# Head pairs of a windowed attention, re-timed between the products of a dense layer

## The chip, the cores and the metric

The kernel runs on one core of a Trainium2 chip. The metric is the device time of one execution in microseconds. Five instruction streams run side by side and meet only at semaphores: PE (matrix products), ACT (ScalarE), DVE (VectorE), POOL (GpSimd) and SP, which issues loads and stores. Each stream is executed in the order in which it is written. An instruction that waits therefore holds everything behind it on its own engine.

## The reference

```python
scores = scale * q @ k.T                      # B=4, H=8, S=768, D=64
keep = (key < 4) | ((0 <= row - key) & (row - key < 128))
a = softmax(where(keep, scores, -1e9));  x = (a @ v) as [3072, 512]
h = x @ w_in;  x2 = (h - tanh(h)) @ w_out     # 512 -> 2048 -> 512
logits = x2 @ w_gate + modality_bias[modality_id]
e = argmax(logits);  g = softmax(logits)[e]   # 8 experts
out = g * (relu(x2 @ w1[e]) @ w2[e])          # 512 -> 1024 -> 512
```

## The kernel before, in words

Every large product is made from two float16 parts of each operand, hi and lo: lo·hi + hi·lo + hi·hi, summed in PSUM. The hi part is written by ACT as a scaled copy, the lo part by DVE or POOL as the difference.

**Units.** The 3072 tokens are 8 chunks of 384. A *pair* r is one block of 128 query rows for two heads: 12 pairs a chunk, 96 in all. Three consecutive pairs (t = 0, 1, 2) belong to the same heads and form a group g; their results share one PSUM tile, `x_out`. The pair t = 0 of an even chunk has fewer keys (132 columns, not 260) and no values product of its own.

**The stages of a pair**, each a function that emits its part on each engine:

- `score_pair`: PE writes the scores of two heads into two banks `s_ps` (L571); DVE adds the mask, writes `probs` and takes the negated row maximum in the same pass (L582); ACT takes the exponential with the row sum (L589). `probs` is a ring of two pairs.
- `normalise`: DVE adds 1e-9 and inverts the row sums (L602, L603); ACT scales into `normed` (L609).
- `gather_sinks` (only t = 2): DVE copies the sink columns of the six normalised tiles into `sinks`.
- `transpose_probs`: PE transposes `normed` into the bank `pt_ps` (L641); ACT copies `pt_hi` (L646), DVE makes `pt_lo` (L650). `transpose_sinks` (only t = 2) sends the sinks through the same bank `pt_ps` (L664, L669, L673).
- `weigh_values`: PE adds the values products to `x_out` (L707), and for t = 2 the sinks' product (L709). The first of a group waits until `x_out` of the group before has been copied out by
- `split_x` (only t = 2): ACT `xt_hi` (L729), DVE `xt_lo` (L732).

**The dense layer.** For chunk m and block f of 16: `mlp_in` (PE, 12 products of 384 columns into the single bank `h_ps`, L752), tanh on ACT (L764), the gate on DVE (L773), then `g_hi` on ACT (L783) and `g_lo` on DVE (L793), and `mlp_out` (PE, 9 products of 512 columns into three banks, L808).

**The order.** `alone` first runs 14 pairs with nothing of the dense layer beside them, together with loads, the scaling and splitting of q, k and v (`conversions`, `prepare_alone`) and the splitting of the weights. Then come 8 windows w, one for each chunk of the dense layer, of 32 *slots* k. An even slot holds `mlp_in` of the next block, an odd one `mlp_out` of this block. Pairs are scored in even slots, inside `mlp_in` (`between`), by the table `plan_slots`. The later stages follow by their age in slots: `ago(2)` is the pair that was scored two slots ago. Before the change transposes come at age 2, inverse and normalising at age 1, sinks at age 3, the values products at age 3 (odd slot, t = 0 and 1) or 4 (even slot, t = 2), and `split_x` at age 5. The split of v for the next batch, scales and weight splits are called at given slots in `prepare`; the routing of the chunk before in `gate_slot`. It borrows the scores' bank, and whoever writes that bank next waits for its last reader (`claim_scores`).

After window 7 the experts' blocks run (L1858, L1909). The change does not touch them.

## Time and profile before

| | us |
|---|---|
| device time, median of three | 1101.09 (1100.54 to 1101.55) |
| the profiled execution's own time | 1097.37 |
| its span in the trace | 1095.8 |
| `alone`, to the first `mlp_out` | 0 to 97 |
| windows 0 to 7 | 97 to 801 |
| experts' blocks | 801 to 1096 |

The page gives for each engine its busy time as a share of the span. The stretches above are cut at the dense layer's products with `w_out`; the rows further down give the same for some stretches. PE's busy time contains its waits only where no product is under way, so the length of a stretch less PE's busy time is the time in which PE does nothing. The windows differ in work: windows 0, 2 and 4 carry the split of v for the next batch, window 0 also the last splits of the weights, and window 7 has no pairs.

### The profile page before, as it was taken

To read this page: it belongs to the slowest core of one execution; us is meant where nothing else is said; L and a number is where in the kernel's file an instruction comes from. 1 tells how busy PE (TensorE), PEld (TensorE's weight loads), DVE (VectorE), ACT (ScalarE), POOL (GpSimd) and SP (SyncE) were. 2 spreads that over 40 slices of the span, in tenths; PEclk is the share of its full clock that TensorE was granted. 3 is DMA by queue.
4 is the path that set the end of the run, shared out by engine and by line. 5 is a ranking of instruction groups with operands and counts; after the bars stand their busy time and mean duration, and the time that the engine had idled before them with its cause. 6 is when DMAs were issued, how large, how long until landed. Compare 5 with 4: busy or idle time off the path is not lost.

```text
span 1095.8 us, 23839 instructions
## 1 busy us (share of the span) xinstructions
PE 995.6 (91%) x7968; PEld 605.7 (55%) x7968; DVE 651.0 (59%) x2272; ACT 581.4 (53%) x1329; POOL 328.7 (30%) x462
## 2 busy tenths in 40 slices
PE   2647889999899999989999989999999999999996
PEld 1524445554455455545455545555477777677774
DVE  6565777657767757766766774655765334543331
ACT  3676687656667656655766664645532223532221
POOL 5675676111224311213321121011024223222222
PEclk9857999999999999999999999999999999999999
DMA  8710000200300211110030020014023411211111
GB/s 301 256 34 19 18 22 32 106 18 18 64 17 19 47 76 36 10 55 18 18 65 18 18 47 2 1 40 173 1 30 104 150 47 48 53 30 52 45 53 42
DMA packets 24375, 60.30 MB, mean 55 GB/s; under 512 B 9504, under 2 KB 9760, under 8 KB 22752
## 3 DMA queue, kind: packets, MB, share of 16 engines
q1 hardware_dynamic: 15392, 45.77, 14.2%
q0 software_dynamic: 5728, 13.43, 3.9%
q8 instruction: 45, 0.74, 0.3%
q10 hardware_dynamic: 3168, 0.02, 0.1%
q14 instruction: 42, 0.34, 0.1%
HBM read 45.35 MB, written 14.12 MB: 54 GB/s over the span
## 4 chain that ended last, share of the span: by engine, by line
PE 63%; DVE 14%; issue 9%; ACT 8%; DMA 3%; DVEq 1%; POOL 1%; ACTq 0%; POOLq 0%; SPq 0%
PE h_ps L752 17%; PE acc L808 14%; PE pt_ps L1858 4%; PE s_ps L1858 4%; PE acc L1909 4%; PE h_ps L1909 4%; PE pt_ps L641 4%; PE s_ps L571 2%; PE x_out L707 2%; ACT probs L589 2%; DVE g_raw L773 2%; DVE pt_lo L650 2%; ACT normed L609 2%; PE s_ps L859 2%; ACT pt_hi L646 1%
## 5 line engine op out<-in xcount | busy, mean ns | idle before, releaser
L808 PE MATMUL acc<-w_out_all,g_hi 128*128 128x512 f16 x768 | 228.4, 379 | 0.0
L752 PE MATMUL h_ps<-xt_hi,w_in_all 128*128 128x384 f16 x960 | 197.7, 329 | 11.5 <-DVE g_raw L773 11.5
L808 PE MATMUL acc<-w_out_all,g_lo 128*128 128x512 f16 x384 | 145.6, 379 | 3.0 <-DVE g_lo L793 2.7
L764 ACT ACTIVATE g_raw<-h_ps,batch_scale 128x384 f32<-128x384 f32 x120 | 69.7, 581 | 117.3 <-PE h_ps L752 113.4
L752 PEld LDWEIGHTS h_ps<-xt_hi,w_in_all 128*128 128x128 f16 x960 | 88.4, 100 | 71.3 <-issue 15.5
L793 DVE SCALAR_TENSOR_TENSOR g_lo<-g_raw,batch_scale,g_hi 128x384 f16<-128x384 f32 x128 | 90.4, 706 | 50.8 <-ACT g_hi L783 50.6
L808 PEld LDWEIGHTS acc<-w_out_all,g_hi 128*128 128x128 f16 x768 | 75.1, 98 | 80.3
L783 ACT ACTIVATE g_hi<-g_raw,batch_scale 128x384 f16<-128x384 f32 x128 | 78.3, 612 | 68.5 <-DVE g_raw L773 66.8
L101 POOL TENSOR_TENSOR tick<-tick 1x1 f32<-1x1 f32 x83 | 15.6, 189 | 314.3 <-DVE payload L931 128.1
L650 DVE TENSOR_TENSOR pt_lo<-pt_ps,pt_hi 128x512 f16<-128x512 f32 (+1 forms) x96 | 62.1, 647 | 68.9 <-ACT pt_hi L646 58.3
L752 PE MATMUL h_ps<-xt_lo,w_in_all 128*128 128x384 f16 x480 | 99.0, 329 | 0.0
L589 ACT ACTIVATE probs<-probs,neg_max 128x260 f32<-128x260 f32 (+1 forms) x192 | 92.0, 482 | 9.7 <-DVE neg_max L582 9.7
L582 DVE CUSTOM_DVE_ANT_0 probs<-s_ps,mask 128x260 f32<-128x260 f32 (+1 forms) x192 | 70.0, 401 | 45.1 <-issue 36.4
L646 ACT ACTIVATE pt_hi<-pt_ps 128x512 f16<-128x512 f32 (+1 forms) x96 | 53.6, 558 | 72.8 <-PE pt_ps L641 72.8
L609 ACT ACTIVATE normed<-probs,row_sum 128x260 f32<-128x260 f32 (+1 forms) x192 | 83.1, 480 | 11.0 <-DVE row_sum L602 10.9
L773 DVE SCALAR_TENSOR_TENSOR g_raw<-h_ps,batch_scale,g_raw 128x384 f32<-128x384 f32 x120 | 73.8, 615 | 23.3 <-ACT g_raw L764 21.6
L641 PE MATMUL pt_ps<-ident,normed 128*128 128x128 f32 x352 | 62.1, 298 | 17.1 <-ACT normed L609 10.2
L450 POOL TENSOR_TENSOR q_lo<-qk_raw,q_hi 128x384 f16<-128x384 f32 x31 | 28.3, 914 | 128.5 <-ACT q_hi L446 128.5
L1822 ACT ACTIVATE xg<-xg,x_scale 128x512 f32<-128x512 f32 x23 | 16.6, 722 | 93.6 <-DVE x_undo L1819 93.6
L752 PEld LDWEIGHTS h_ps<-xt_lo,w_in_all 128*128 128x128 f16 x480 | 47.4, 99 | 31.9 <-issue 1.3
L429 POOL TENSOR_SCALAR qk_raw<-qk_raw,qk_scale 128x384 f32<-128x384 f32 (+2 forms) x62 | 40.1, 659 | 75.7 <-DVE qk_scale L420 75.7
L641 PEld LDWEIGHTS pt_ps<-ident,normed 128*128 128x128 f32 x352 | 40.1, 148 | 39.4 <-issue 21.1
(315 smaller groups left out, 2093.9 us busy)
## 6 DMA issues: line engine op xcount, KB each, us to landing
qk_raw<-in_qk SPq DMA_DIRECT2D x31, 454.0 KB, 3.3
raw<-in_w SPq DMA_DIRECT2D x16, 512.0 KB, 8.4
v_raw<-in_v SPq DMA_DIRECT2D x4, 1536.0 KB, 8.2
x_tokens<-x SPq DMA_DIRECT2D x24, 256.0 KB, 4.7
w_in_all<-in_w_in SPq DMA_DIRECT2D x4, 1024.0 KB, 9.7
w_out_all<-in_w_out SPq DMA_DIRECT2D x4, 1024.0 KB, 9.3
x_tokens<-g_raw SPq DMA_DIRECT2D x1, 1024.0 KB, 12.2
vs_raw<-in_v SPq DMA_DIRECT2D x24, 4.0 KB
```

The costliest lines, as they stand in the source:

```text
L582: eng.tensor_tensor_reduce(out=probs[:, r % RING, j, cols], in0=s_banks[j][:, cols], in1=m, scale=-SCALE, scalar=3.0e38, op0=ALU.add, op1= ...
L589: eng.activation(x, x, ACT.Exp, bias=neg_max[:, r % RING, j:j + 1], scale=-1.0, accum_out=row_sum[:, r % RING, j:j + 1]).then_inc(q["exped ...
L609: eng.activation(normed[:, 2 * t + j, cols], probs[:, r % RING, j, cols], ACT.Copy, scale=total)\
L641: mm = eng.transpose(out[:, j, b - first, :], normed[:, 2 * t + j, b * KB:b * KB + P], ident[:])
L650: eng.tensor_tensor(at(pt_lo), out, at(pt_hi), ALU.subtract).then_inc(q["pt_lo_done"], 1)
L752: mm = eng.matmul(h_of(m, f), w16[0][:, f, x * DM + k * P:x * DM + (k + 1) * P], r[:, par, k, :], start=(i == 0), stop=(i == 3 * KD - 1))
L773: eng.scalar_tensor_tensor(g, h_of(m, f), batch_scale[:, b, 0:1], g, ALU.mult, ALU.subtract).then_inc(q["g_done"], 1)
L783: eng.activation(g_hi[f % 2][:], g, ACT.Copy, scale=batch_scale[:, b, 1:2]).then_inc(q["g_hi_done"], 1)
L793: eng.scalar_tensor_tensor(g_lo[f % 2][:], g, batch_scale[:, b, 1:2], g_hi[f % 2][:], ALU.mult, ALU.subtract)\
L808: mm = eng.matmul(acc[t][:, :], l[f % 2][:, t * P:(t + 1) * P], w16[1][:, f, x * DM:(x + 1) * DM], start=(f == 0 and i == 0), stop=(f == N ...
L1858: mm = eng.matmul(hid_ps[c][:, (f - 4 * c) * P:(f - 4 * c + 1) * P], w[:, k, f * P:(f + 1) * P], x[p][:, k * P:(k + 1) * P], start=(i == 0 ...
L1909: mm = eng.matmul(y_ps[bank][:, :], l[:, f * P:(f + 1) * P], rhs, start=(f == 0 and i == 0), stop=(f == KF - 1 and i == 2))
```

## The change

- **Values products** (`weigh_values`): the last argument goes; all three pairs of a group are done at age 4, at the end of an even slot, after `mlp_in`. None is left at the end of an odd slot.
- **Free slots** (`plan_slots`): in window 0 slots 8, 16, 24 (10, 20, 30 before), in the others 6, 14, 22, 30 (4, 10, 16, 26 before). With 14 pairs in `alone` each free slot then stands right behind a pair t = 2. The last pair is scored in slot 20 of window 6, not 22.
- **Odd slots on ACT**: `split_x` first, then `mlp_split` (`g_hi`), sinks, and `normalise` last. On DVE: gate, `split_x`, `normalise`, `g_lo`, sinks.
- **Routing** (`gate_slot`), but for window 7: transposes in slots 6, 10, 14 (4, 10, 16), logits two slots later, choice from 17 (20), rank from 22 (26).
- **Batch of v**: maxima in slots 1, 3, 7, 7, 9, 11 (0 to 5), scale in slot 15 (9), the six multiplications in 16 to 21 and the six splits in 17 to 22, one a slot (every second slot from 10 and 12), the sinks' multiplication in 23.
- **`conversions`**: the maxima of q and k at 6g−9 and 6g−7 (6g−10 and 6g−9), both odd, the scale with the second.
- **`alone`**: scores of the next pair are issued right after the transposes on PE, and right after `normalise` on DVE, ahead of v's maxima, scale chains and `split_x`. v's maxima leave the startup; v's splits and the sinks come one or two half-steps later. Values products all run two pairs behind.
- **`sink_halves`** on POOL waits in batch 1 for `qk_mult` instead of `w_lo1`.

```diff
-                if b == 1:
-                    eng.wait_ge(q["w_lo1"], 14)
-                if b >= 2:
+                if b:
                     eng.wait_ge(q["qk_mult"], 2 * (2 * HP * b + 1))
...
-        def weigh_values(E, eng, r, last):
+        def weigh_values(E, eng, r):
...
-            if E == "pe" and last == (t == TPC - 1) and not is_first(r):
+            last = t == TPC - 1
+            if E == "pe" and not is_first(r):
...
-            if k in (4, 10, 16):
...
+            late = g == NC - 2
+            turns = (4, 10, 16) if late else (6, 10, 14)
+            chooses, ranks = (20, 27) if late else (17, 22)
...
-                tops = (1, 1, 1) if g == 1 else (6 * g - 10, 6 * g - 9, 6 * g - 8)
-                splits = (3, 4) if g == 1 else (6 * g - 5, 6 * g - 3)
+                tops = (1, 1, 1) if g == 1 else (6 * g - 9, 6 * g - 7, 6 * g - 7)
+                splits = (2, 3) if g == 1 else (6 * g - 5, 6 * g - 3)
...
-            if i < 2:
-                v_tops(E, eng, 0, 2 * i + 2)
-                v_tops(E, eng, 0, 2 * i + 3)
-            if i == 1:
+            if i in (0, 2):
+                for blk in range(TPC):
+                    v_tops(E, eng, 0, TPC * (i // 2) + blk)
+            if i == 2:
...
-            if i in (1, 2, 3):
-                v_split(E, eng, 0, i - 1)
-            if i == 2:
+            if i in (2, 3, 4):
+                v_split(E, eng, 0, i - 2)
+            if i == 4:
                 sink_multiply(E, eng, 0)
-            if i == 4:
+            if i == 5:
                 sink_halves(E, eng, 0)
...
-                if k < NB2:
-                    v_tops(E, eng, b, k)
-                if k == NB2 and E == "dve":
+                for blk in {1: (0,), 3: (1,), 7: (2, 3), 9: (4,), 11: (5,)}.get(k, ()):
+                    v_tops(E, eng, b, blk)
+                if k == 11 and E == "dve":
                     spread(E, eng, v_spread(b))
-                if k == 10:
+                if k == 15:
+                    v_scales(E, eng, b)
+                if 16 <= k < 22:
+                    v_multiply(E, eng, b, k - 16)
+                if 17 <= k < 23:
+                    v_split(E, eng, b, k - 17)
+                if k == 23:
                     batch_scales(E, eng, b)
-                if 10 <= k < 22 and k % 2 == 0:
-                    v_multiply(E, eng, b, (k - 10) // 2)
-                if 12 <= k < 24 and k % 2 == 0:
-                    v_split(E, eng, b, (k - 12) // 2)
-                if k == 22:
                     sink_multiply(E, eng, b)
...
+            if E in ("pe", "dve"):
+                score_pair(E, eng, 0)
             for r in range(ALONE):
                 if E == "pe":
-                    stage(score_pair, E, eng, r)
                     stage(transpose_probs, E, eng, r - 1)
-                    stage(weigh_values, E, eng, r - 2, True)
+                    if r + 1 < ALONE:
+                        score_pair(E, eng, r + 1)
+                    stage(weigh_values, E, eng, r - 2)
...
                 if E == "dve":
-                    stage(score_pair, E, eng, r)
                     stage(gather_sinks, E, eng, r - 1)
                     stage(transpose_probs, E, eng, r - 1)
+                    normalise(E, eng, r)
+                    if r + 1 < ALONE:
+                        score_pair(E, eng, r + 1)
+                    stage(split_x, E, eng, r - 2)
+                    stage(transpose_sinks, E, eng, r - 1)
                 prepare_alone(E, eng, 2 * r)
...
-                    if k not in ((10, 20, 30) if w == 0 else (4, 10, 16, 26)):
+                    if k not in ((8, 16, 24) if w == 0 else (6, 14, 22, 30)):
...
                     if not even:
                         mlp_out(E, eng, w, f, between)
-                        stage(weigh_values, E, eng, ago(3), False)
                     else:
                         if nxt:
                             mlp_in(E, eng, *nxt, between)
-                        stage(weigh_values, E, eng, ago(4), True)
+                        stage(weigh_values, E, eng, ago(4))
...
                     else:
+                        stage(split_x, E, eng, ago(5))
                         if nxt:
                             mlp_split(E, eng, *nxt)
+                        stage(transpose_sinks, E, eng, ago(3))
                         stage(normalise, E, eng, ago(1))
-                        stage(transpose_sinks, E, eng, ago(3))
-                        stage(split_x, E, eng, ago(5))
```

Three places in the order of the instructions. In the changed kernel the same lines have numbers one or two lower.

PE at the start of window 2, before. `x_out` 128x384 is the sinks' product that ends a group, `x_out` 64x128 begins the next group.

```order
L709 MATMUL x_out<-pt_hi,vs_all 128x384
L808 MATMUL acc<-w_out_all,g_lo 128x512
L808 MATMUL acc<-w_out_all,g_hi 128x512 x2
L808 MATMUL acc<-w_out_all,g_lo 128x512
L808 MATMUL acc<-w_out_all,g_hi 128x512 x2
L808 MATMUL acc<-w_out_all,g_lo 128x512
L808 MATMUL acc<-w_out_all,g_hi 128x512 x2
L707 MATMUL x_out<-pt_lo,v_hi 64x128 x2
L707 MATMUL x_out<-pt_hi,v_lo 64x128 x2
L707 MATMUL x_out<-pt_hi,v_hi 64x128 x2
```

The same place now:

```order
L807 MATMUL acc<-w_out_all,g_lo 128x512
L807 MATMUL acc<-w_out_all,g_hi 128x512 x2
L751 MATMUL h_ps<-xt_hi,w_in_all 128x384 x4
L751 MATMUL h_ps<-xt_lo,w_in_all 128x384 x4
L569 MATMUL s_ps<-k_hi,q_lo 128x260 x2
L569 MATMUL s_ps<-k_lo,q_hi 128x260 x2
L569 MATMUL s_ps<-k_hi,q_hi 128x260 x2
L639 MATMUL pt_ps<-ident,normed 128x128 x4
L751 MATMUL h_ps<-xt_hi,w_in_all 128x384 x4
L706 MATMUL x_out<-pt_lo,v_hi 64x128 x2
L706 MATMUL x_out<-pt_hi,v_lo 64x128 x2
L706 MATMUL x_out<-pt_hi,v_hi 64x128 x2
```

Before, the first product of the next group stands one `mlp_out` behind the end of the last group. Now a whole slot of `mlp_in` (with its scores and transposes) and more stands between them, and the product comes behind an `mlp_in`.

DVE in `alone`, at the pairs 10 and 11, before. `pt_lo` is of pair 10, `row_sum` of pair 11, `qk_exp` to `qk_scale` is the scale chain of a group of q and k.

```order
L650 TENSOR_TENSOR pt_lo<-pt_ps,pt_hi 128x2x256
L412 TENSOR_SCALAR qk_exp<-qk_top 128x1
L414 TENSOR_SCALAR qk_exp<-qk_exp 128x1
L412 TENSOR_SCALAR qk_exp<-qk_top 128x1
L414 TENSOR_SCALAR qk_exp<-qk_exp 128x1
L416 TENSOR_SCALAR qk_half<-qk_exp 128x1
L418 TENSOR_SCALAR qk_half<-qk_half 128x1
L419 TENSOR_SCALAR qk_scale<-qk_half 128x1
L420 TENSOR_SCALAR qk_scale<-qk_scale 128x1
L602 TENSOR_SCALAR row_sum<-row_sum 128x1
```

The same place now; `probs` is of pair 12.

```order
L648 TENSOR_TENSOR pt_lo<-pt_ps,pt_hi 128x2x256
L600 TENSOR_SCALAR row_sum<-row_sum 128x1
L601 RECIPROCAL row_sum<-row_sum 128x1
L600 TENSOR_SCALAR row_sum<-row_sum 128x1
L601 RECIPROCAL row_sum<-row_sum 128x1
L578 MEMSET tick 1x1
L580 ISA probs,neg_max<-s_ps,mask 128x260
L580 ISA neg_max 128x1
L580 ISA probs,neg_max<-s_ps,mask 128x260
L580 ISA neg_max 128x1
L401 TENSOR_REDUCE qk_top<-qk_raw 128x1
L412 TENSOR_SCALAR qk_exp<-qk_top 128x1
```

The chain of eight small operations stood between `pt_lo` and the inverse; it now stands behind the scores of the next pair, together with one of the maxima (`qk_top`).

ACT in window 0 where v is split (`v_hi`), before:

```order
L507 ACTIVATE v_hi<-v_raw 128x4x2x64
L783 ACTIVATE g_hi<-g_raw,batch_scale 128x384
L609 ACTIVATE normed<-probs,row_sum 128x260 x2
L669 ACTIVATE pt_hi<-pt_ps 128x384
L357 ACTIVATE w_in_all<-w_in_all,w_scale 128x512
L446 ACTIVATE q_hi<-qk_raw 128x384
L646 ACTIVATE pt_hi<-pt_ps 128x2x256
L764 ACTIVATE g_raw<-h_ps,batch_scale 128x384
L589 ACTIVATE probs,row_sum<-probs,neg_max 128x260 x2
L507 ACTIVATE v_hi<-v_raw 128x4x2x64
```

The same place now:

```order
L507 ACTIVATE v_hi<-v_raw 128x4x2x64
L446 ACTIVATE q_hi<-qk_raw 128x384
L644 ACTIVATE pt_hi<-pt_ps 128x2x256
L763 ACTIVATE g_raw<-h_ps,batch_scale 128x384
L587 ACTIVATE probs,row_sum<-probs,neg_max 128x260 x2
L507 ACTIVATE v_hi<-v_raw 128x4x2x64
L782 ACTIVATE g_hi<-g_raw,batch_scale 128x384
L607 ACTIVATE normed<-probs,row_sum 128x260 x2
L357 ACTIVATE w_out_all<-w_out_all,w_scale 128x512
L507 ACTIVATE v_hi<-v_raw 128x4x2x64
```

Before, ten instructions lie from one `v_hi` to the next, the two included. Now three splits of v stand in these ten rows.

## Rows read from the trace of the kernel before

**Rows 1.** Page, part 1: busy time, share of the span and instructions of each engine.

```profile
PE 995.6 (91%) x7968; PEld 605.7 (55%) x7968; DVE 651.0 (59%) x2272; ACT 581.4 (53%) x1329; POOL 328.7 (30%) x462
```

**Rows 2.** Busy time by stretch: stretch, length, each engine's busy us (instructions), clock, DMA.

```profile
0.00:97.00 97.00, 48.92 (x387) 30.96 (x388) 55.94 (x257) 54.67 (x142) 60.59 (x87) 0.79 0.48 172
97.00:195.00 98.00, 86.82 (x599) 46.02 (x597) 72.32 (x244) 72.90 (x170) 63.70 (x73) 1.00 0.07 21
195.00:282.00 87.00, 84.80 (x569) 46.61 (x568) 58.55 (x227) 53.63 (x137) 16.21 (x20) 1.00 0.16 45
282.00:376.00 94.00, 87.10 (x599) 47.90 (x597) 66.81 (x243) 59.21 (x145) 29.56 (x34) 1.00 0.14 30
...
801.00:1096.00 295.00, 280.08 (x3135) 208.27 (x3133) 119.78 (x343) 89.49 (x148) 81.92 (x152) 1.00 0.20 61
```

**Rows 3.** Waits of PE, 97 to 195 us: total us, times, longest us.

```profile
PE x_out L707 <- issue: 5.0, 3, 2.5
PE h_ps L752 <- DVE g_raw L773: 2.8, 4, 1.1
PE pt_ps L641 <- DVE pt_hi L673: 2.5, 4, 0.9
```

**Rows 4.** Waits of PE, 195 to 731 us.

```profile
PE x_out L707 <- issue: 10.6, 9, 2.2
PE h_ps L752 <- DVE g_raw L773: 7.1, 18, 0.9
PE pt_ps L641 <- DVE pt_hi L673: 4.4, 9, 0.6
```

**Rows 5.** Timeline of PE, 286 to 293 us: start, us, instruction, [idle before, releaser].

```profile
286.33 0.63 PE L641 MATMUL pt_ps<-ident,normed 128*128 128x128 f32 x4 [0.50 <-DVE pt_hi L673]
...
289.84 0.59 PE L808 MATMUL acc<-w_out_all,g_hi 128*128 128x512 f16 x2
292.67 0.25 PE L707 MATMUL x_out<-pt_lo,v_hi 128*64 128x128 f16 x2 [2.23 <-issue]
```

**Rows 6.** Timeline of DVE, the same stretch.

```profile
292.01 0.56 DVE L732 SCALAR_TENSOR_TENSOR xt_lo<-x_out,xt_hi 128x384 f16<-128x384 f32 x1 [0.56 <-ACT xt_hi L729]
```

**Rows 7.** Waits of ACT, 18 to 89 us.

```profile
ACT normed L609 <- DVE row_sum L602: 9.8, 8, 2.0
...
ACT probs L589 <- DVE neg_max L582: 5.2, 6, 1.6
```

**Rows 8.** Timeline of DVE, 75 to 78 us.

```profile
75.70 0.14 DVE L412 TENSOR_SCALAR qk_exp<-qk_top 128x1 int32<-128x1 int32 x1
...
77.14 0.14 DVE L602 TENSOR_SCALAR row_sum<-row_sum 128x1 f32<-128x1 f32 x1
```

**Rows 9.** Timeline of POOL, 27 to 30.4 us.

```profile
27.46 1.15 POOL L534 TENSOR_TENSOR vs_all<-vs_raw,vs_all 32x512 f16<-32x512 f32 x1 [0.43 <-ACT vs_all L524]
28.71 0.70 POOL L492 TENSOR_SCALAR v_raw<-v_raw,v_scale 128x512 f32<-128x512 f32 x1
29.37 0.94 POOL L450 TENSOR_TENSOR k_lo<-qk_raw,k_hi 128x396 f16<-128x396 f32 x1
```

**Rows 10.** Timeline of PE, 30 us.

```profile
30.36 0.23 PE L571 MATMUL s_ps<-k_hi,q_lo 64*128 64x132 f16 x2 [0.76 <-POOL k_lo L450]
```

**Rows 11.** Timeline of DVE, 16.7 us.

```profile
16.72 0.29 DVE L331 TENSOR_REDUCE row_top<-acc 128x1 f32<-128x128 f32 x1 [0.95 <-PE acc L324]
```

**Rows 12.** Timeline of ACT, 322 us.

```profile
322.31 0.62 ACT L507 ACTIVATE v_hi<-v_raw 128x512 f16<-128x512 f32 x1
```

**Rows 13.** Line 793 on DVE, 97 to 195 us, then 195 to 282 us: ns min/median/max.

```profile
L793 DVE SCALAR_TENSOR_TENSOR g_lo<-g_raw,batch_scale,g_hi x16: 619/1039/1504, 101.7 to 191.7; 128x384 f16<-128x384 f32 x16
...
L793 DVE SCALAR_TENSOR_TENSOR g_lo<-g_raw,batch_scale,g_hi x16: 617/618/619, 196.3 to 279.3; 128x384 f16<-128x384 f32 x16
```

**Rows 14.** Timeline of POOL, then DVE, 323 us.

```profile
323.00 1.16 POOL L510 TENSOR_TENSOR v_lo<-v_raw,v_hi 128x512 f16<-128x512 f32 x1 [9.03 <-ACT v_hi L507]
...
323.46 1.11 DVE L793 SCALAR_TENSOR_TENSOR g_lo<-g_raw,batch_scale,g_hi 128x384 f16<-128x384 f32 x1 [0.67 <-ACT g_hi L783]
```

More of the change, by code:

```diff
@@ L943, in gate_slot @@
         def gate_slot(E, eng, g, k):
-            if k in (4, 10, 16):
-                gate_transpose(E, eng, g, (k - 4) // 6)
-            if k in (6, 12, 18):
-                gate_logits(E, eng, g, (k - 6) // 6)
-            if 20 <= k < 25:
-                gate_choose(E, eng, g, (k - 20,))
-            at = 27 if g == NC - 2 else 26
-            if at <= k < at + 4:
-                gate_rank(E, eng, g, (k - at,))
+            late = g == NC - 2
+            turns = (4, 10, 16) if late else (6, 10, 14)
+            chooses, ranks = (20, 27) if late else (17, 22)
+            if k in turns:
+                gate_transpose(E, eng, g, turns.index(k))
+            if k - 2 in turns:
+                gate_logits(E, eng, g, turns.index(k - 2))
+            if chooses <= k < chooses + 5:
+                gate_choose(E, eng, g, (k - chooses,))
+            if ranks <= k < ranks + 4:
+                gate_rank(E, eng, g, (k - ranks,))
         def prepare_expert(E, eng, k):
@@ L1128, in startup @@
             conv(E, eng, 0, 0, 1)
-            v_tops(E, eng, 0, 0)
-            v_tops(E, eng, 0, 1)
             for s in range(2):
@@ L1170, in prepare_alone @@
                 weight_gram(E, eng, 0, i - 4)
-            if i in (4, 6, 8):
-                v_multiply(E, eng, 0, i // 2 + 1)
-            if i in (5, 7, 9):
-                v_split(E, eng, 0, (i + 1) // 2)
+            if i in (6, 8, 10):
+                v_multiply(E, eng, 0, i // 2)
+            if i in (7, 9, 11):
+                v_split(E, eng, 0, (i - 1) // 2)
             if i == 8:
@@ L1224, in before_slot @@
                 gate_slot(E, eng, w - 1, k)
-            if w % 2 == 0 and w < NC - 2 and k == 9:
-                b = w // 2 + 1
-                if E == "pe":
-                    spread(E, eng, v_spread(b))
-                v_scales(E, eng, b)
+            if w % 2 == 0 and w < NC - 2 and k == 15 and E == "pe":
+                spread(E, eng, v_spread(w // 2 + 1))
         def stage(work_on, E, eng, r, *more):
@@ L1235, in alone @@
         def alone(E, eng):
+            if E in ("pe", "dve"):
+                score_pair(E, eng, 0)
             for r in range(ALONE):
                 if E == "pe":
-                    stage(score_pair, E, eng, r)
                     stage(transpose_probs, E, eng, r - 1)
-                    stage(weigh_values, E, eng, r - 2, True)
+                    if r + 1 < ALONE:
+                        score_pair(E, eng, r + 1)
+                    stage(weigh_values, E, eng, r - 2)
                 if E == "act":
-                    stage(score_pair, E, eng, r)
+                    score_pair(E, eng, r)
                     stage(transpose_probs, E, eng, r - 1)
@@ L1255, in alone @@
                     stage(transpose_sinks, E, eng, r - 1)
-                    stage(weigh_values, E, eng, r - 1, False)
                 if E == "act":
                     stage(transpose_sinks, E, eng, r - 1)
-                    stage(normalise, E, eng, r)
-                if E == "dve":
-                    stage(normalise, E, eng, r)
-                    stage(split_x, E, eng, r - 2)
-                    stage(transpose_sinks, E, eng, r - 1)
+                    normalise(E, eng, r)
                 prepare_alone(E, eng, 2 * r + 1)
@@ L1323, in window @@
                             mlp_gate(E, eng, *nxt)
+                        stage(split_x, E, eng, ago(5))
                         stage(normalise, E, eng, ago(1))
@@ L1327, in window @@
                         stage(transpose_sinks, E, eng, ago(3))
-                        stage(split_x, E, eng, ago(5))
                 if w == NC - 1:
```

1 line of the change is left out of this document (removed).

## The prediction

> **What bounds the kernel now.** I read the page first, then busy time by stretch, then what PE waited for in each stretch, then the timelines around the longest waits. PE is busy for 995.6 us of the span [rows 1]. The stretches split the rest [rows 2]: `alone` has 97 − 48.9 = 48.1 us in which PE does nothing, window 0 98 − 86.8 = 11.2, window 1 2.2, window 2 6.9, and the experts' part, which no edit reaches, 14.9. So there are two kinds of place. In the windows PE is the bound and only its waits can be won. In `alone` PE is idle half the time, and a chain that runs from DVE to ACT and back sets the pace of the pairs.
>
> PE's waits in the windows with pairs are three kinds [rows 3, 4]: before the values products 5.0 + 10.6 = 15.6 us, before transposes (the bank `pt_ps` is still read for the sinks) 2.5 + 4.4 = 6.9, and before `mlp_in` (the single bank `h_ps`) 2.8 + 7.1 = 9.9. The first is put down to "issue", so I looked at its longest. PE's last `mlp_out` product starts at 289.84, then PE stands for 2.23 us until 292.67 [rows 5]; DVE's `xt_lo` of the group before ends at 292.01 + 0.56 = 292.57 [rows 6]. The wait is the one for `x_out` to be copied out.
>
> **The values products and the free slots, in the windows.** At age 4, and with a free slot behind each third pair, the first product of a group comes at age 8 counted from the scores of the pair that ended the group before, while `split_x` is written at age 5. Three slots lie between, and the pt parts of a pair are made at age 2. I take all 15.6 us off. The sinks' transposes go through `pt_ps` at age 3, and the transposes that used to follow at age 4 now find a free slot there in steady state. I take the 6.9 us off too. PE's work is the same, only its place moves. At the bank `h_ps` the count of PE instructions between one `mlp_in` and the next stays the same for a pair (values before `mlp_out` instead of behind it), so the 9.9 us stay. Sum of what goes: 22.5 us.
>
> What comes new in the windows:
>
> - v's scale in slot 15: PE's spread writes the scores' bank, and the logits of slot 16 may write it only when DVE has read it. That read is 0.29 us in the one place that I looked at [rows 11], but it stands in DVE's slot behind the gate, `g_lo` and the sinks. I take 0.7 us late, in windows 2 and 4 (window 0 has no routing): 1.4 us. From below it is 0, if DVE is ahead; from above 2.2, the longest wait of PE in these windows [rows 4], each time.
> - The transposes of the routing in slot 10 stand in a slot with scores, in six windows. Their copy on ACT has two thirds of an `mlp_in` to finish before the scores need the bank. I take 0, at most 0.6 each (about a `v_hi` of ACT, which copies as many elements [rows 12]).
> - The six splits of v come one a slot in windows 0, 2 and 4. ACT does 0.62 us for each [rows 12], POOL 0.70 for the multiplication [rows 9] and 1.16 for the difference [rows 14]. The 18 splits are the same work, but in a slot pair ACT now has 1.24 us of it, not 0.62. ACT is busy 74% of window 0 (72.9 of 98) and 63% of window 2 (59.2 of 94) [rows 2], so the surplus fits in windows 2 and 4 on average and hardly in window 0, which has the weights as well. I take 0.6 us a slot pair for three slot pairs, 1.8, in window 0 and half of that in each of windows 2 and 4: 3.6 us together. From below 0 (all hidden), from above each split holds PE by its 0.62: 18 × 0.62 = 11.2.
>
> A rule bears on this last item. In the trace `g_lo` takes 618 ns in window 1, where POOL has little to do, but a median of 1039 in window 0 [rows 13], and 1.11 us where it meets POOL's `v_lo` [rows 14]. The Trainium skill (Advanced Engine Details and Errata, Miscellaneous Facts: GPSIMD and DVE Details) has it that POOL and DVE share a read and a write interface, and that an operation of DVE with two operands in SBUF conflicts with POOL's. The trace agrees for `g_lo`, which reads two. By the rule denser POOL work costs DVE up to 0.5 us for each of the 18 `v_lo`, 9 us if PE waited for each; without it the sum stays as above. Before the change every `v_lo` was issued for an even slot and already met a `g_lo` in the odd one, so I add nothing.
>
> Windows: 22.5 − 1.4 − 3.6 = 17.5 us won.
>
> **`alone`.** Between 18 and 89 us ACT waited 9.8 us for inverted row sums and 5.2 us for the maxima [rows 7], 15.0 in all, in a chain in which ACT's own work is the other part. The scale chain of q and k takes 77.14 − 75.70 = 1.44 us on DVE and stands right before the row sums [rows 8], once in three pairs, so 4 times from pair 2 on: 5.8 us. It now stands behind the scores of the next pair, while ACT has two exponentials and a `pt_hi` to do. The maxima's waits (5.2) go where DVE's other work held the scores back; they are now written directly behind the inverse. Against that, DVE's work is only moved: the gap behind the scores must take scale chain and maximum together (over 2 us), and `pt_lo` stands behind it. I take half of 5.8 + 5.2, that is 5.5, less 0.5 for pair 9, where the scale of the weights falls in the same gap: 5.0 us.
>
> At the start pair 3 waits for POOL's `k_lo` [rows 10]. Before it POOL did the sinks' part (1.15) and a multiplication (0.70) [rows 9], which now stand behind it: 1.85 us, about 2. That v's scale comes later on DVE works against it; that the first scores no longer wait for v's maxima, for it.
>
> `alone`: 5 + 2 = 7 us won. From below −2: POOL is busy 60.6 of the 97 us [rows 2] and its order could hold the start back as before, with the denser gap coming on top. From above 13: all of 5.8 + 5.2 and the 2.
>
> **Sum.** 17.5 + 7 = 24.5 us. The profiled execution took 1097.37 us (span 1095.8, 1.6 around it), so the changed kernel would take 1072.9 in such an execution. The median of the runs shown is 3.7 us above that execution; at their level it is 1101.1 − 24.5 = 1076.6, and I say 1076.
>
> **The rivals.**
>
> 1. *`alone` gains nothing* (15%). For it: ACT's order in `alone` is nearly the same, and POOL and ACT are each busy well over half of it [rows 2]. Against it: two of DVE's jobs leave the chain. Time: 1101.1 − 17.5 = 1083.6.
> 2. *The splits of v clog ACT* (13%). Each of the 18 holds PE by about 0.62 us, 11.2 instead of 3.6, and in `alone` the moved work comes back as a later `pt_lo` (gain 2). 22.5 − 1.4 − 11.2 + 2 = 11.9: 1089. For it: rows 12 and 13. Against it: half the splits now stand in odd slots.
> 3. *More than I take* (10%): the waits for `h_ps` go as well (half of 9.9, since DVE no longer comes to the gate late from pairs that were held by PE), and `alone` gives 11. 24.5 + 5 + 4 = 33.5: 1067.6.
> 4. *Slower, by POOL's queue* (5%). ACT's split of v waits for POOL's multiplication, which stands behind POOL's difference for the split before, and in window 0 behind those of weights. If POOL lags by a slot, every one of the 18 splits keeps ACT, and so PE, for a POOL round of 0.70 + 1.16 = 1.86 us: 33.5 us against 24.5 + 3.6 = 28.1 won. Time: 1106.5. It decides from 28.1 / 18 = 1.56 us a split. Against it: POOL is busy only 29.6 of 94 us in window 2 [rows 2].
>
> The forecast has 53%. About 0.2% (2 us) is what a measurement can tell from no change. Rivals 1 to 3 are all faster; between 4 and them I leave 3% for no change and 1% more for slower: faster 0.91, same 0.03, slower 0.06.
>
> The range must hold the forecast, rivals 1 and 3 and most of 2. Terms at their bounds: everything won and nothing new gives 22.5 + 13 = 35.5, 1065.6; the dear ends of `alone` and of the splits together 22.5 − 4.4 − 3.6 − 11.2 − 2 = 1.3, which needs all of them at once. I say 1065 to 1092.
>
> **What will show it.** PE's waits before values products between the first `mlp_out` and the last pair should fall from 15.6 us to under 2, those before transposes from 6.9 to under 2, those before `mlp_in` stay near 10. The first `mlp_out` should start at 90 to 91 us instead of 97. In windows 2 and 4 a wait of under 1 us before the logits of slot 16 should be new. ACT's waits for row sums in `alone` should fall to about half; DVE should wait less before `pt_lo`. The experts' part should keep its 295 us. I am wrong if waits before transposes or `mlp_in` grow by what the others lose, if windows 0, 2 and 4 gain less than 1, 3 and 5 despite their larger waits, or if the stretch before 97 us keeps its length.

## The result, and the profile after

The changed kernel took 1074.24 us (median of four, 1072.89 to 1075.87), the kernel before beside it 1100.82 us. The ratio is 0.976 (95%: 0.974 to 0.978), 2.4% faster. The forecast was 1076. The profiled execution took 1072.89 us, its span is 1071.3, against 1097.37 and 1095.8 before.

Cut at the first and last product with `w_out`, in us:

| | before | after | won | predicted |
|---|---|---|---|---|
| `alone` | 97.5 | 94.6 | 2.9 | 7 |
| windows | 703.7 | 680.8 | 22.9 | 17.5 |
| experts | 294.6 | 295.9 | −1.3 | 0 |
| span | 1095.8 | 1071.3 | 24.5 | 24.5 |

So the sum is right, but its two large terms are off in opposite directions, `alone` by 4 us and the windows by 5. The page's part 1, of the changed kernel:

```profile
PE 993.2 (93%) x7968; PEld 607.1 (57%) x7968; DVE 649.5 (61%) x2272; ACT 581.6 (54%) x1329; POOL 327.6 (31%) x462
```

Its busy time by stretch, with the columns of [rows 2]:

```profile
0.00:94.00 94.00, 47.57 (x383) 30.62 (x384) 55.81 (x257) 54.79 (x143) 60.76 (x87) 0.80 0.49 178
94.00:182.00 88.00, 82.60 (x559) 42.81 (x556) 64.41 (x221) 67.82 (x162) 61.59 (x71) 1.00 0.06 20
182.00:270.00 88.00, 86.57 (x597) 48.42 (x596) 62.46 (x243) 57.05 (x144) 17.79 (x23) 1.00 0.15 52
270.00:360.00 90.00, 87.45 (x601) 48.30 (x600) 67.26 (x243) 59.45 (x146) 29.27 (x34) 1.00 0.12 31
...
775.00:1071.00 296.00, 282.87 (x3136) 210.32 (x3134) 120.15 (x343) 89.33 (x148) 82.02 (x152) 0.98 0.20 60
```

Against [rows 2] every engine has the same work to do; only the stretches are shorter. Windows 0, 2 and 4 gain 10, 4 and 6 us by these cuts, windows 1, 3 and 5 gain −1, 2 and 2. The larger waits were in the former, so this sign of being wrong did not show. Window 2 was 94 long with 6.9 us in which PE did nothing, and is now 90 with 2.5. What PE waited for in the changed kernel, 94 to 705 us (all windows with pairs; total, times, longest):

```profile
PE pt_ps L662 <- DVE pt_lo L648: 8.1, 9, 1.2
PE s_ps L858 <- DVE row_top L331: 1.4, 2, 0.7
PE h_ps L751 <- DVE g_raw L772: 1.4, 3, 0.6
PE pt_ps L639 <- ACT normed L607: 1.3, 1, 1.3
```

Beside [rows 3, 4]: the waits before values products (15.6) are gone, and so are those of the pairs' transposes (6.9). The waits before `mlp_in`, which I had standing at 9.9, are 1.4. New are 8.1 us before L662, the *sinks'* transposes, and the 2 × 0.7 us before the logits of slot 16. The timeline of window 2 shows both halves, DVE first:

```profile
333.70 0.75 DVE L792 SCALAR_TENSOR_TENSOR g_lo<-g_raw,batch_scale,g_hi 128x384 f16<-128x384 f32 x1 [0.18 <-ACT g_hi L782]
334.36 0.56 DVE L401 TENSOR_REDUCE qk_top<-qk_raw 128x1 f32<-128x396 f32 x1
334.95 0.15 DVE L412 TENSOR_SCALAR qk_exp<-qk_top 128x1 int32<-128x1 int32 x1
...
336.33 0.15 DVE L420 TENSOR_SCALAR qk_scale<-qk_scale 128x1 int32<-128x1 int32 x1
336.40 0.56 DVE L920 TENSOR_TENSOR counts<-s_ps,counts 128x8 f32<-128x8 f32 x3
336.99 0.18 DVE L921 TENSOR_TENSOR work<-s_ps,counts 128x24 f32<-128x24 f32 x1
337.20 0.59 DVE L619 COPY sinks<-normed 128x72 f32<-128x72 f32 x1
337.72 0.67 DVE L648 TENSOR_TENSOR pt_lo<-pt_ps,pt_hi 128x512 f16<-128x512 f32 x1
338.31 0.59 DVE L923 TENSOR_TENSOR work<-work,region 128x24 f32<-128x24 f32 x1
338.93 0.63 DVE L924 TENSOR_TENSOR work<-work,chosen 128x24 f32<-128x24 f32 x1
339.59 0.62 DVE L772 SCALAR_TENSOR_TENSOR g_raw<-h_ps,batch_scale,g_raw 128x384 f32<-128x384 f32 x1
```

And PE in the same stretch:

```profile
338.53 0.52 PE L662 MATMUL pt_ps<-ident,sinks 128*128 128x128 f32 x3 [0.85 <-DVE pt_lo L648]
...
340.27 0.82 PE L751 MATMUL h_ps<-xt_hi,w_in_all 128*128 128x384 f16 x4 [0.57 <-DVE g_raw L772]
```

Maximum and scale chain (334.36 to 336.5) now stand at the end of an odd slot. What comes late is `pt_lo`, behind the chain, the first steps of the routing's rank (L920, L921) and the sinks' copy, and with it the bank `pt_ps`. The gate is still late here, by 0.57 us, and this is the longest of the three waits before `mlp_in` that are left.

### The profile page after: what moved, and what is told of

It reads as the page before. It is cut to its first block, busy times and chain, and to the rows that moved or that the text cites. A ratio compares the mean times of both kernels' runs of the same rounds, so it can differ in the third digit from the quotient of the medians.

```text
span 1071.3 us, 23847 instructions
## 1 busy us (share of the span) xinstructions
PE 993.2 (93%) x7968; PEld 607.1 (57%) x7968; DVE 649.5 (61%) x2272; ACT 581.6 (54%) x1329; POOL 327.6 (31%) x462
## 4 chain that ended last, share of the span: by engine, by line
PE 74%; DVE 11%; ACT 6%; issue 5%; POOL 2%; DVEq 1%; DMA 0%; ACTq 0%; SPq 0%; POOLq 0%
PE h_ps L751 18%; PE acc L807 18%; PE s_ps L1856 6%; PE h_ps L1907 6%; PE pt_ps L1856 6%; PE acc L1907 5%; PE pt_ps L639 3%; PE s_ps L569 3%; PE x_out L706 2%; ACT probs L587 1%; PE s_ps L858 1%; DVE pt_lo L648 1%; DVE qk_top L401 1%; PE pt_ps L662 1%; PE x_out L1833 1%
## 5 line engine op out<-in xcount | busy, mean ns | idle before, releaser
L751 PEld LDWEIGHTS h_ps<-xt_hi,w_in_all 128*128 128x128 f16 x960 | 91.2, 100 | 62.3 <-issue 7.0
L792 DVE SCALAR_TENSOR_TENSOR g_lo<-g_raw,batch_scale,g_hi 128x384 f16<-128x384 f32 x128 | 84.7, 662 | 44.5 <-ACT g_hi L782 44.5
L429 POOL TENSOR_SCALAR qk_raw<-qk_raw,qk_scale 128x384 f32<-128x384 f32 (+2 forms) x62 | 37.7, 621 | 125.2 <-DVE qk_scale L420 125.0
L807 PEld LDWEIGHTS acc<-w_out_all,g_lo 128*128 128x128 f16 x384 | 37.5, 98 | 41.1 <-issue 6.2
```

The lines of the kernel that those rows point to most:

```text
L751: mm = eng.matmul(h_of(m, f), w16[0][:, f, x * DM + k * P:x * DM + (k + 1) * P], r[:, par, k, :], start=(i == 0), stop=(i == 3 * KD - 1))
L792: eng.scalar_tensor_tensor(g_lo[f % 2][:], g, batch_scale[:, b, 1:2], g_hi[f % 2][:], ALU.mult, ALU.subtract)\
L807: mm = eng.matmul(acc[t][:, :], l[f % 2][:, t * P:(t + 1) * P], w16[1][:, f, x * DM:(x + 1) * DM], start=(f == 0 and i == 0), stop=(f == N ...
```

## The experiments

Times are medians of five executions (six for the maxima put back, twelve for values and free slots alone). The lengths are those of one profiled execution each: span, `alone`, windows and tail as in the table above. The ratio is to the kernel before (1097.9, 1098.5 and 1098.0 us in the three groups of runs).

**The changed kernel again**, as the base for the others.

> The changed kernel once more, as the base for the three kernels that run with it. Expected: 24.5 to 27 us under the kernel before, the first product with w_out at 94 to 95 us, PE's idle time in the windows 18 us as in its first profile.

1073.64 us, ratio 0.978 (0.975 to 0.981); 1072.2 = 94.8 + 680.7 + 296.7. The windows repeat to 0.1 us, `alone` and tail less well; so I read the windows from the traces.

**Values of t = 0 and 1 back at age 3**, in odd slots of the windows, on the changed kernel.

```diff
                     if not even:
                         mlp_out(E, eng, w, f, between)
+                        weigh_aged(E, eng, ago(3), False)
...
-                        stage(weigh_values, E, eng, ago(4))
+                        weigh_aged(E, eng, ago(4), True)
...
+            weigh_values(E, eng, ALONE - 2)
```

`weigh_aged` calls `weigh_values` for t = 2 when its last argument is true, otherwise for t = 0 and 1.

> The changed kernel, but in the windows the values products of t = 0 and 1 stand again at age 3 at the end of an odd slot. Theory 1 (the wait for x_out was the start of a group right behind the end of the last; the free slot behind each third pair alone puts four slots between, so age 4 adds nothing to it): the first product of a group comes at age 7, split_x at age 5, no wait for x_out comes back; the kernel is within 2 us of the changed one. Theory 2 (my prediction's wording: age 4 is what takes the wait off): waits before values products of 5 us or more come back and the kernel is 5 to 10 us slower. Waits before mlp_in: theory 1 leaves them near 1.5 us in the windows; if the place of the values products is what emptied them, they return to 5 to 9.

1078.59 us, 0.982 (0.979 to 0.984); windows 683.9. Back at age 3 the windows are 3.2 us longer, between what the two theories said. The waits before values products do not return (0.5 us); the wait that grows is that of the sinks' transposes, 12.3 us.

**Free slots and the routing's slots as before.**

```diff
-            turns = (4, 10, 16) if late else (6, 10, 14)
-            chooses, ranks = (20, 27) if late else (17, 22)
...
+            if k in (4, 10, 16):
...
-                    if k not in ((8, 16, 24) if w == 0 else (6, 14, 22, 30)):
+                    if k not in ((10, 20, 30) if w == 0 else (4, 10, 16, 26)):
```

> The changed kernel with the free slots and the routing's slots of before (free 10, 20, 30 in window 0, else 4, 10, 16, 26). Theory 1 (the free slots carry most of the windows' gain): waits before transposes at the bank of the sinks come back (4 to 7 us) and with them part of those before values products, where a group follows at once: 8 to 14 us slower. Theory 2 (the order in the odd slots and age 4 carry it): under 4 us slower.

1079.77 us, 0.983 (0.981 to 0.986); windows 686.0, of which about 1.6 us may be a granted clock of 0.96 over 40 us in window 0 (150 to 190 us; an estimate, 4% of 40). So 3.6 to 5.3 us, again as waits at L662 (12.2 us, 16 times), none before values products. With the rest of the change in place, either measure is enough to remove the 15.6 us of waits that the prediction had credited to the two together.

**`alone` as before** (values products two pairs behind, as in the changed kernel).

```diff
-            if E in ("pe", "dve"):
-                score_pair(E, eng, 0)
             for r in range(ALONE):
                 if E == "pe":
+                    stage(score_pair, E, eng, r)
                     stage(transpose_probs, E, eng, r - 1)
-                    if r + 1 < ALONE:
-                        score_pair(E, eng, r + 1)
...
+                    stage(normalise, E, eng, r)
...
```

> The changed kernel with the order of alone as before (scores at the head of a step, maxima of v in the startup, splits of v and sinks a step earlier), values products still two pairs behind. The first profile says that this part won 2.9 us, where I had predicted 7. Theory 1 (POOL's k_lo now sets the pace and eats the rest): 2 to 4 us slower than the changed kernel, waits of PE for k_lo under 2 us, waits of ACT for row sums and maxima back near 15 us. Theory 2 (the part is worth nothing or costs; the 2.9 us are from elsewhere): within 1 us or faster.

1075.91 us, 0.981 (0.978 to 0.984); `alone` 96.6, windows 680.7. By this pair of traces the new `alone` is worth 1.8 us; the timed medians differ by 2.3 with overlapping intervals. Both are far below the 7, and 1.8 is within what the first `mlp_out` moves between traces of the same code (see the seam, below).

**Odd slots of ACT and DVE in the old order.**

```diff
-                        stage(split_x, E, eng, ago(5))
                         if nxt:
                             mlp_split(E, eng, *nxt)
-                        stage(transpose_sinks, E, eng, ago(3))
                         stage(normalise, E, eng, ago(1))
+                        stage(transpose_sinks, E, eng, ago(3))
+                        stage(split_x, E, eng, ago(5))
...
```

The cut shows ACT; DVE's `split_x` goes to its end in the same way.

> The changed kernel with the order in the odd slots as before: on ACT g_hi, normalise, sinks, split_x; on DVE gate, normalise, g_lo, sinks, split_x. Theory 1 (with a free slot behind each group nothing waits for split_x, so its place is free): within 2 us of the changed kernel. Theory 2 (normalise last on ACT is what emptied the waits before transposes and mlp_in): 4 to 8 us slower, with waits before mlp_in back at 5 us or more.

1071.58 us, 0.976 (0.973 to 0.978); windows 679.2. The new order gains nothing: undone, the windows are 1.6 us shorter.

**v's batch in its old slots.**

```diff
-                if 17 <= k < 23:
-                    v_split(E, eng, b, k - 17)
+                if 12 <= k < 24 and k % 2 == 0:
+                    v_split(E, eng, b, (k - 12) // 2)
...
```

> The changed kernel with the batch of v at its slots of before (maxima in 0 to 5, scale in 9, splits every second slot from 12 to 22). My prediction took 1.4 us for the scale in slot 15 and 3.6 us for the six splits in a row. Theory 1 (that is right): waits before the logits of slot 16 are gone (1.4 us in the profile), and 1 to 5 us are won. Theory 2 (the new slots are what lets DVE keep up, because the maxima no longer stand in front of the scores of the first slots): 2 to 6 us lost, with new waits in the first slots of windows 0, 2 and 4.

1071.56 us, 0.975 (0.972 to 0.978); windows 678.3, 2.5 us shorter, and the waits for `row_top` before the logits are gone (1.4 us); the waits for `x2t` rise from 0.5 to 1.2. I had priced scale and splits at 5.0.

**Part 0 of the rank behind `pt_lo`** on DVE, to test what the new wait at L662 is.

```diff
-            if ranks <= k < ranks + 4:
+            if ranks <= k < ranks + 4 and (late or E != "dve" or k != ranks):
...
+                        if k == 22 and 1 <= w < NC - 1:
+                            gate_rank(E, eng, w - 1, (0,))
```

> The changed kernel, but in slot 22 of windows 1 to 6 DVE does the first part of the rank behind pt_lo, not ahead of it. The new wait of 0.85 to 0.97 us before the sinks' transposes in slot 23 (windows 1 to 5) should be DVE's pt_lo held up by that part. Theory 1: that wait is gone, 3.5 to 4.8 us won. Rival: pt_lo is late for another reason (ACT's pt_hi behind normalise); the wait stays and nothing moves, or the rank's own steps come late and hold back the scores of slot 24.

1071.73 us, 0.976 (0.973 to 0.979); windows 679.0. The wait at L662 falls from 8.1 to 3.5 as it should, but that before `mlp_in` rises from 1.4 to 4.7 (longest 1.6): of 4.6 us taken from one wait the next took 3.3, and the windows are 1.8 us shorter, not 3.5 to 4.8. In this slot the order on DVE mostly chooses which bank is late.

**Conversions first** in `alone` from pair 3 on, which puts POOL's `k_lo` ahead of the weights' work.

```diff
-                prepare_alone(E, eng, 2 * r)
-                conversions(E, eng, 2 * r)
+                for work in (conversions, prepare_alone) if r >= 3 else (prepare_alone, conversions):
+                    work(E, eng, 2 * r)
...
```

> The changed kernel, but in alone, from pair 3 on, the conversions of q and k stand ahead of the weights' splits in each half-step. In the changed kernel PE waits 8.2 us in four waits for POOL's k_lo. Theory 1 (POOL's order is what limits alone): the waits for k_lo after 50 us (3.6 and 1.3) fall to under 1, and the windows start 2 to 4 us earlier. Rival (POOL's total is the limit, or ACT's chain): the waits move to the weights or to normalise, and the start moves by under 1 us.

1072.57 us, 0.976 (0.974 to 0.979); `alone` 92.6 in the profile, PE's waits for `k_lo` 5.8 us in place of 8.2. The two waits after 50 us were to fall to under 1; the longer of them is still 2.1, for 3.6. The timed medians differ by 1.1 us with overlapping ranges, so the 2 us of the trace are not established.

The first eight runs left the 22.9 us unexplained: undoing values or free slots gives back 3 to 5 each. The next two build the change up from the kernel before, and a third puts one line back.

**Values products and free slots alone**, on the kernel before.

```diff
-                    if k not in ((10, 20, 30) if w == 0 else (4, 10, 16, 26)):
+                    if k not in ((8, 16, 24) if w == 0 else (6, 14, 22, 30)):
...
-                        stage(weigh_values, E, eng, ago(3), False)
...
-                        stage(weigh_values, E, eng, ago(4), True)
+                        r = ago(4)
+                        if r is not None and r >= ALONE - 1:
+                            stage(weigh_values, E, eng, r, r % TPC == TPC - 1)
```

> The kernel before with two parts alone, both in the windows: values products at age 4 for all pairs, and the free slots with the routing's slots. Undoing either of them from the changed kernel brought no wait for x_out back. Theory 1 (these two are enough for x_out and for the sinks' bank): the waits before values products, 15.6 us, are gone, the windows take 703.7 − 15 − 3 = about 686 us, while the waits before mlp_in (9.9) stay, since nothing else has moved. Rival: the order of the odd slots (split_x first) is needed too; 3 us or more of waits for x_out remain. Rival for mlp_in: its waits fall under 3 us already here.

1094.60 us, 0.996 (0.994 to 0.998): 0.4%, where my sum had 22.5 us for it. Windows 701.9 (some 1.5 of that may be a granted clock of 0.95 over 30 us in window 0; an estimate, 5% of 30). PE's waits, 97 to 731 us:

```profile
PE h_ps L752 <- DVE g_raw L773: 24.4, 27, 2.0
PE s_ps L571 <- ACT x2t L849: 1.4, 2, 0.7
...
PE pt_ps L641 <- ACT normed L609: 0.2, 1, 0.2
```

Both named kinds of wait are gone, and the wait before `mlp_in` has grown from 9.9 to 24.4. PE's idle time in the windows fell by 6.0 us (37.4 to 31.4) and their length by 1.8; 1.5 of the difference may be the clock, the rest stays open (ends of matmuls are modelled). The timeline of this kernel in window 2 shows one of the longest of these waits, DVE and POOL:

```profile
340.87 0.69 DVE L650 TENSOR_TENSOR pt_lo<-pt_ps,pt_hi 128x512 f16<-128x512 f32 x1 [0.30 <-ACT pt_hi L646]
...
341.47 0.14 DVE L412 TENSOR_SCALAR qk_exp<-qk_top 128x1 int32<-128x1 int32 x1
...
342.84 0.15 DVE L420 TENSOR_SCALAR qk_scale<-qk_scale 128x1 int32<-128x1 int32 x1
342.91 0.17 DVE L894 TENSOR_REDUCE den<-expd 128x3 f32<-128x24 f32 x1
343.05 1.15 POOL L510 TENSOR_TENSOR v_lo<-v_raw,v_hi 128x512 f16<-128x512 f32 x1 [1.85 <-ACT v_hi L507]
343.11 1.12 DVE L895 TENSOR_SCALAR den<-den 128x3 f32<-128x3 f32 x1
...
344.48 0.62 DVE L773 SCALAR_TENSOR_TENSOR g_raw<-h_ps,batch_scale,g_raw 128x384 f32<-128x384 f32 x1
```

PE there:

```profile
340.78 0.25 PE L707 MATMUL x_out<-pt_lo,v_hi 128*64 128x128 f16 x2
...
345.15 0.66 PE L752 MATMUL h_ps<-xt_hi,w_in_all 128*128 128x384 f16 x3 [1.93 <-DVE g_raw L773]
```

The scale chain (341.47 to 342.9) and a part of the routing stand right ahead of the gate, and the gate is what `mlp_in` waits for. The kernel before has the chain in the same place. DVE of that kernel, in window 2:

```profile
372.60 0.15 DVE L420 TENSOR_SCALAR qk_scale<-qk_scale 128x1 int32<-128x1 int32 x1
372.67 0.61 DVE L773 SCALAR_TENSOR_TENSOR g_raw<-h_ps,batch_scale,g_raw 128x384 f32<-128x384 f32 x1
```

And PE:

```profile
371.93 0.30 PE L707 MATMUL x_out<-pt_lo,v_hi 128*64 128x256 f16 x2
...
373.34 0.82 PE L752 MATMUL h_ps<-xt_hi,w_in_all 128*128 128x384 f16 x4 [0.88 <-DVE g_raw L773]
```

Gone through for all 26 chains of the windows, the two traces say more. In the kernel before, 9.0 of the 9.9 us before `mlp_in` (20 of 22 waits) come behind a gate with the chain ahead of it; in this one it is some 20 of the 24.4. Two things around the chain have changed. The first is the work of PE between the two `mlp_in` on either side of such a gate: before, it had six values products of 256 columns there in 19 of the 26 places and none in 7; with all values at age 4 it has six of 128 columns in 13 and none in 13. By the starts in these rows that is about 4 us less work in which DVE could catch up (an estimate). The second is that in five places the moved routing stands between chain and gate; the waits there add up to 8.0 us, for 2.8 in the kernel before. The rest of the growth stays open.

**The same with the maxima and the scale chain at ends of odd slots** (from the fifth group on, so that `alone` stays as it was; `sink_halves` waits as in the changed kernel).

```diff
-                tops = (1, 1, 1) if g == 1 else (6 * g - 10, 6 * g - 9, 6 * g - 8)
+                tops = (1, 1, 1) if g == 1 else (6 * g - 9, 6 * g - 7, 6 * g - 7) if g > HP else (6 * g - 10, 6 * g - 9, 6 * g - 8)
```

> As the kernel before it, and the maxima and scale chain of q and k (from group 5 on) at the ends of odd slots, 6g−9 and 6g−7, as in the changed kernel. Theory 1: what made DVE late at the gate, and so PE before mlp_in, was this chain (1.4 us with its eight steps) at the end of an even slot, right ahead of the gate; the waits before mlp_in fall from 9 us to under 3 and the windows take 6 to 8 us less than with the two parts alone, 679 to 681 us. Rival: they stay above 6 us and the maxima of v or the odd order carry that.

1072.95 us, 0.977 (0.974 to 0.979): the whole gain of the change, with `alone`, the odd slots' order and the batch of v all as they were before. Windows 681.3, 20.6 us less than without (19 without the clock's 1.5), where I had expected 6 to 8. PE's waits, 94 to 731 us:

```profile
PE pt_ps L662 <- DVE pt_lo L648: 7.7, 10, 1.2
PE h_ps L750 <- DVE g_raw L771: 2.8, 6, 0.6
```

The wait before `mlp_in` falls from 24.4 to 2.8, and the sinks' transposes take 7.7 of it.

**The changed kernel with the maxima alone put back.**

```diff
-                tops = (1, 1, 1) if g == 1 else (6 * g - 9, 6 * g - 7, 6 * g - 7)
+                tops = (1, 1, 1) if g == 1 else (6 * g - 9, 6 * g - 7, 6 * g - 7) if g <= HP else (6 * g - 10, 6 * g - 9, 6 * g - 8)
```

> The changed kernel with the maxima and scale chain of q and k as before (6g−10, 6g−9, 6g−8) from group 5 on, that is in the windows alone. Theory 1 (the chain ahead of the gate): waits before mlp_in rise from 1.4 to 6 us or more and the windows are 4 to 8 us longer. Rival: within 2 us.

1087.66 us, 0.990 (0.988 to 0.992); windows 695.4, 14.6 longer than with them moved and not 4 to 8. PE's waits, 95 to 731 us:

```profile
PE h_ps L751 <- DVE g_raw L772: 18.0, 24, 1.9
PE x_out L706 <- DVE pt_hi L671: 1.5, 1, 1.5
```

PE's idle time in the windows is 9.1 us above that of the changed kernel (27.3 for 18.2); the other 5.5 us of the 14.6 stand in its modelled busy time and stay open. So one line of the change carries 14 us (1087.7 against 1073.6, from two groups of runs whose kernels before agree to 0.1) from one side and 19 to 21 from the other. Not run were the maxima alone on the kernel before. The waits that they could remove there come to about 9 us, so the 19 to 21 are in part the cost of the two parts without the maxima: the gain belongs to the parts together.

**A better version**: conversions first, rank late, ACT's and DVE's old order and v's old slots, all on the changed kernel. Its edits are the four diffs above.

> The changed kernel with four things put together: conversions of q and k ahead of the weights' splits in alone from pair 3 on, first part of the rank behind pt_lo in slot 22, and the odd order and the batch of v as before. In the windows the three took 1.7, 1.5 and 2.4 us less than the changed kernel by their profiles. If they add: windows 675 us, alone 2 us shorter, the kernel 5 to 8 us under the changed one, 1066 to 1069. Rival (they share the same waits before the sinks' transposes and mlp_in): 1070 to 1072, no better than each alone.

1069.10 us, 0.973 (0.970 to 0.975), faster than either kernel: 1067.4 = 93.7 + 677.8 + 295.9. PE's waits, 94 to 705 us:

```profile
PE h_ps L751 <- DVE g_raw L772: 6.2, 8, 1.7
PE pt_ps L662 <- DVE pt_lo L648: 2.3, 5, 0.9
PE s_ps L569 <- ACT x2t L848: 1.4, 2, 0.7
```

The singles promised 1.6 + 2.5 + 1.8 in the windows, 5.9; together they gave 3.0 (680.8 to 677.8). `alone` is 0.9 us shorter than in the changed kernel's first trace, where 2 were expected.

## Why the prediction was right, and where it was not

**Waits before values products, 15.6 us off: the waits went, the time did not follow.** They are at zero in the changed kernel, but taken away with the free slots and little else they are worth 1.8 to 3.3 us. It would be easy to say that DVE had worked off its chain while PE stood before `x_out`. The trace of the kernel before does not bear this out: in none of its 12 stands there does the chain run, and the next one begins 4 to 11 us later (292.67 and 301.95 in window 2). The step that failed reads "the count of PE instructions between one `mlp_in` and the next stays the same for a pair (values before `mlp_out` instead of behind it), so the 9.9 us stay". The count is the same over a whole group, but not at the gates behind the chain, where 9.0 of the 9.9 us were: there the products of a pair t = 1 gave way to those of a pair t = 0, which are half as many columns or none. And the 9.9 us did not stay: they grew to 24.4 with values and free slots alone, and fell to 1.4 with the chain moved too. I had written down the sign that would refute me (waits before `mlp_in` "grow by what the others lose"). The changed kernel does not show it; the run with values and free slots alone does for the larger part, 14.5 us of the 22.5 that the others lose.

**A term I left out.** The moved maxima of q and k and the eight-step chain, 0.55 + 1.44 us on DVE, I priced in `alone` and not at all in the windows, where they stand ahead of the gate in every group. With the values products and the free slots moved they are worth 14 to 21 us of the windows. Rows 8 held the duration, and the list of the change held the move; missing was the question of what stands in the same DVE slot ahead of L773.

**Transposes, 6.9 to under 2: half right.** The pairs' transposes wait 1.3 us in all. For the sinks' transposes themselves I took no wait, and they wait 8.1 us for `pt_lo` of the same pair through the one bank `pt_ps`. That is one wait handed on again: the run with the late gate has none of it, and once the gate is early it is 7.7.

**v's scale, 1.4 us:** measured 2 × 0.7 = 1.4, as taken. **The splits, 3.6:** undoing the batch gives 2.5 with the scale in it, so about 1.1; rival 2 falls. **Routing in slot 10, 0:** the waits for `x2t` are 0.5 us. **The odd slots' order** I gave no price; it costs 1.6. Each of these three is a single part undone, and such figures do not add up here.

**`alone`, 7 us: mis-sized, 2.9 in the profile and 1.8 by its own run.** The first `mlp_out` starts at 94.6, not at 90 to 91. The two waits of [rows 7] did shrink, more than I took. ACT's waits, 18 to 82 us:

```profile
ACT v_hi L507 <- POOL v_raw L492: 10.4, 1, 10.4
ACT pt_hi L667 <- PE pt_ps L662: 8.0, 4, 3.2
...
ACT normed L607 <- DVE row_sum L600: 2.6, 5, 0.7
...
ACT probs L587 <- DVE neg_max L580: 0.7, 1, 0.7
```

From 9.8 to 2.6 and from 5.2 to 0.7, 11.7 us less, while those for `v_hi` rose from 3.8 to 10.4 and those for the sinks' transposes from 5.5 to 8.0. The 2 us at the start came: pair 3 begins at 28.02 for 30.36 [rows 10]. But pair 13 is only 3.3 us sooner by its maxima (80.0 for 83.3), so the 5 us that I had put on the later pairs are about 1. PE's waits, 18 to 86 us:

```profile
PE pt_ps L639 <- ACT normed L607: 11.1, 8, 3.8
PE s_ps L569 <- POOL k_lo L450: 8.2, 4, 3.6
```

With the old `alone` put back, the waits for `k_lo` were 3.4 us in this stretch. The longest one, PE and then POOL:

```profile
56.30 1.16 POOL L363 TENSOR_TENSOR w_in_all<-w_in_all 128x512 f16<-128x512 f32 x1
57.41 0.94 POOL L450 TENSOR_TENSOR k_lo<-qk_raw,k_hi 128x396 f16<-128x396 f32 x1
...
58.41 0.29 PE L569 MATMUL s_ps<-k_hi,q_lo 64*128 64x132 f16 x2 [3.59 <-POOL k_lo L450]
```

Moving `k_lo` ahead shortens this gap to 2.10. My lower bound named this ("its order could hold the start back"), but I took half of the two waits where about a tenth was right: ACT waits for other things instead. Rival 1 (nothing won) was the nearer story for `alone`, and by the scatter described next the runs do not rule it out: its 1083.6 missed because the windows gave more.

**Clock at the seam.** With the changed kernel's code of `alone` the first product with `w_out` lay between 94.1 and 98.2 us, with that of the kernel before at 97.5, 96.6 and 94.3. The two overlap, so the traces do not separate the new order of `alone` from this scatter. A stretch at the lower level (1.2 GHz) ends at different moments. In the changed kernel (busy time by stretch) PE's clock is at it until 89 us:

```profile
59.00:89.00 30.00, 18.06 (x98) 9.69 (x99) 18.04 (x88) 19.91 (x51) 22.46 (x26) 0.50 0.10 32
```

With v's old slots it is at it until 98 us:

```profile
67.00:98.00 31.00, 21.07 (x107) 10.31 (x107) 15.01 (x64) 19.00 (x48) 19.32 (x21) 0.51 0.11 31
```

In the second the stretch reaches the first products of the dense layer. What `alone` wins can so be lost again before window 0; what sets the moment these runs do not settle.

**The experts' part** took 295.9 for 294.6; over the runs it lies between 293.8 and 297.5 with no edit there, so the −1.3 is scatter.

In sum: 24.5 forecast, 24.5 measured in the span, with 4 us too much for `alone`, 5 too little for the windows and 1.3 of scatter in the tail, and inside the windows by a mechanism that I had not priced. That the totals agree is chance.

## What to carry to other kernels

A wait in an in-order stream is worth what remains when the next wait for the same late engine is counted. Before crediting one, list what the releasing engine does between two of its releases, and ask which bank comes next if the waiting engine arrives sooner by that much. Look for small work (here 2 us of maximum and scale chain a group) that stands directly ahead of an instruction that frees a single buffer; here moving it, with the products moved, was worth more than moving the products alone. And test a change of many parts from both ends: single undos missed the main part here until the one line that the prediction had not priced was undone.

## What the runs showed of the hardware

Small operations of DVE can take several times their length beside POOL. In the run with values and free slots alone `den` (L895, 128x3) took 1.12 us, starting 0.06 behind POOL's `v_lo` and ending 0.03 behind its end. The same operation in the changed kernel, and the sinks' copy (ns min/median/max), 94 to 705 us:

```profile
L894 DVE TENSOR_SCALAR den<-den x6: 169/170/402, 241.8 to 682.0; 128x3 f32<-128x3 f32 x6
...
L619 DVE COPY sinks<-normed x28: 202/209/695, 101.4 to 685.0; 128x72 f32<-128x72 f32 x28
```

In the changed kernel's timeline of window 2 above, L923 takes 0.59 us beside POOL's `v_lo` (337.70 to 338.86; the median of its six is 0.17), while the int32 chain of L412 to L420 keeps 0.15 to 0.21 a step beside another `v_lo` (335.07 to 336.23) and `pt_lo`, which reads PSUM, its 0.67. `g_lo` in window 0 has a median of 0.73 us for 1.04 before [rows 13]. The Trainium skill (SBUF — State Buffer, SBUF: two separate sides) describes the port pair that DVE and POOL share as a lock held for a whole instruction, with the later one blocked, where DVE's operation is in a two-port mode or has two inputs in SBUF; the 1.12 us that end with `v_lo` agree. Here the operation stood ahead of the gate, for 1.12 us and not 0.17, and PE waited 1.93 us for that gate; so a small operation there can cost PE nearly a whole POOL operation.
